# Second layer's up product by Strassen's seven half-block products, with weight factors made beside the first layer

## What is computed

```
    h = x @ w_in                       # layer one: 2304 x 512 times 512 x 2048
    r = np.maximum(h, 0.0)
    g = s * (r * r) + b
    x = (g @ w_out).astype(np.float32)
    ...
    h = x @ w_in                       # layer two, weights of its own
    g = np.maximum(h, 0.0) + alpha * np.minimum(h, 0.0)
    return (g @ w_out).astype(np.float32)
```

## Time and profile before

| | |
|---|---|
| median of 3 runs | 885.54 us (884.36 to 886.65) |
| the profiled execution, its time | 886.29 us |
| its span, first to last instruction | 884.0 us |
| PE busy | 870.4 us, 98% of the span |
| DVE / ACT / POOL busy | 416.4 / 289.2 / 55.8 us |
| matmuls of layer two | 1152 of 384 columns, 864 of 512 |
| mean granted TensorE clock | 0.996 |

### The profile page before, as it was taken

One profiled execution on the slowest core, in us unless ns is written; L12 is line 12 of the kernel. 1 busy time (PEld: TensorE's weight loads), 2 busy tenths in 40 slices (PEclk: granted clock), 3 DMA queues, 4 the chain that ended last, 5 costly groups with the idle time before them and its releaser, 6 DMA issues.

```text
span 884.0 us, 13811 instructions
## 1 busy us (share of the span) xinstructions
PE 870.4 (98%) x5628; PEld 816.5 (92%) x5628; DVE 416.4 (47%) x986; ACT 289.2 (33%) x727; POOL 55.8 (6%) x54
## 2 busy tenths in 40 slices
PE   6999999999999999999999999999999999999998
PEld 5899999999999999999999999999999999999997
DVE  6666544454444444443454444444444444444443
ACT  6566434344344344433554111111111111111111
POOL 4100000000000000000566000000000000000000
PEclk8999999999999999999999999999999999999999
DMA  7653311111121111201444001001100100100000
GB/s 251 215 161 101 118 60 53 55 66 55 55 66 62 41 55 67 72 1 64 128 127 145 15 1 42 30 1 33 39 1 27 47 0 19 54 1 7 30 1 36
DMA packets 19198, 53.05 MB, mean 60 GB/s; under 512 B 2112, under 2 KB 2112, under 8 KB 19136
## 3 DMA queue, kind: packets, MB, share of 16 engines
q1 hardware_dynamic: 19136, 52.18, 18.2%
HBM read 42.74 MB, written 9.44 MB: 59 GB/s over the span
## 4 chain that ended last, share of the span: by engine, by line
PE 93%; DVE 3%; ACT 3%; issue 0%; DMA 0%; DVEq 0%; ACTq 0%
PE hid L333 44%; PE acc L381 22%; PE acc L371 21%; PE bank_x L402 2%; PE bank_x L393 1%; ACT p L533 1%; PE bank_x L451 1%; PE bank_y L451 1%; ACT p L572 1%; ACT g L518 1%; DVE g L654 1%; DVE relu L640 1%; DVE w_in L664 0%; DVE p L738 0%; ACT w_in L528 0%
## 5 line engine op out<-in xcount | busy, mean ns | idle before, releaser
L333 PE MATMUL hid<-x,w_in 128*128 128x384 f32 (+1 forms) x2316 | 435.2, 336 | 0.0
L333 PEld LDWEIGHTS hid<-x,w_in 128*128 128x128 f32 x2316 | 406.0, 188 | 11.0 <-issue 2.6
L371 PE MATMUL acc<-g,w_out 128*128 128x384 f32 x1152 | 223.6, 337 | 1.1 <-DVE g L654 1.1
L381 PE MATMUL acc<-w_out,g 128*128 128x512 f32 x864 | 215.4, 393 | 0.4 <-DVE g L658 0.4
L371 PEld LDWEIGHTS acc<-g,w_out 128*128 128x128 f32 x1152 | 199.8, 188 | 2.8 <-DVE g L654 1.8
L381 PEld LDWEIGHTS acc<-w_out,g 128*128 128x128 f32 x864 | 160.7, 188 | 30.0 <-DVE g L658 0.8
L521 ACT ACTIVATE g<-relu 128x384 fp32r<-128x384 f32 x96 | 50.5, 526 | 332.2 <-DVE relu L648 332.2
L640 DVE SCALAR_TENSOR_TENSOR relu<-relu,consts 128x384 f32<-128x384 f32 x96 | 66.4, 692 | 152.3 <-ACT relu L508 152.3
L645 DVE TENSOR_SCALAR relu<-hid,consts 128x384 f32<-128x384 f32 x96 | 59.3, 618 | 161.5 <-PE hid L333 161.5
L508 ACT ACTIVATE relu<-hid 128x384 f32<-128x384 f32 x96 | 46.7, 486 | 130.6 <-PE hid L333 130.6
L654 DVE SCALAR_TENSOR_TENSOR g<-relu,consts,g 128x384 fp32r<-128x384 f32 x96 | 59.9, 624 | 57.4 <-ACT g L518 56.2
(11 more groups left out here) (85 smaller groups left out, 355.1 us busy)
## 6 DMA issues: line engine op xcount, KB each, us to landing
...
x_scratch<-outs SPq DMA_DIRECT2D x6, 768.0 KB, 4.1
qk<-x_scratch SPq DMA_DIRECT2D x6, 768.0 KB, 5.9
piece<-in_w_in_a SPq DMA_DIRECT2D x16, 256.0 KB, 2.6
piece<-in_w_out_a SPq DMA_DIRECT2D x16, 256.0 KB, 3.1
piece<-in_w_in_b SPq DMA_DIRECT2D x16, 256.0 KB, 2.8
piece<-in_w_out_b SPq DMA_DIRECT2D x16, 256.0 KB, 2.7
```

The costliest lines, as they stand in the source:

```text
L333: mm = pe.matmul(hid[f % 2][:, at], w_in[:, wi, f, dc, :], x[:, t % 2, xi, dc, at], start=(dc == 0 and n == 0), stop=(dc == ND - 1 and n = ...
L371: mm = pe.matmul(acc[dc][:, 0:TILE], w_out[:, wi, f, dc * 128:(dc + 1) * 128], g[:, f % 2, gi, :], start=(f == 0 and n == 0), stop=(f == N ...
L381: mm = pe.matmul(acc[a][:, :], g[:, f % 2, gi, a * 128:(a + 1) * 128], w_out[:, wi, f, :], start=(f == 0 and n == 0), stop=(f == NF - 1 an ...
```

## The change

Layer two's `up` is computed in passes. A pass k takes a tile of 768 tokens (two of the old ones) and two hidden blocks; there are 3 tiles of 8 passes (NW = 3, PER = 8, NK = 24). Width, tokens and hidden block pair are halved each, and the 8 half-block products become 7 (`multiply(k, n)`, line 494, 6 matmuls of 384 columns each), of sums of weight blocks (7 factors per hidden pair, `ring`) and sums of token blocks (7 per tile, `xc`). Their results are summed to the four quarters of the hidden values.

- **Weight factors.** Beside layer one, in tiles 1 to 4, in 14 of 16 steps: ACT makes a high part of 128 x 256 (`made_high`), DVE the low part (`made_low`) and in 8 of 14 a difference (`made_sum`); SP stores each factor (256 KB) to DRAM (`keep_made`). In layer two SP loads 7 a pass (`load_factor`, four slots) and ACT copies each into `ring` (`keep_factor`, line 740). POOL no longer splits layer two's `w_in`.
- **Token factors.** Once per tile: three sums and one more of 768 columns on DVE (`factor_sums`, `last_sum`), seven high parts on ACT (`factor_high`, line 718) and seven low parts on DVE (`factor_low`), 768 columns each.
- **A pass on DVE and ACT.** ACT copies product 0 (`copy_first`, 747). DVE has 7 `sum_up` (line 1050, PSUM plus SBUF), 4 `leak` of two instructions (lines 1059 and 1061, in SBUF now) and 4 `quarter_low` (line 1066); ACT has 4 `quarter_high` (line 756) and 7 `keep_factor`. All are 384 columns, the factor copies 2 x 256.
- **Down.** `gather(k, n)`, n = 0 to 5: 6 matmuls of 512 columns each, one of six 128-token blocks, as many as before. A pass of PE alternates `multiply(k, n)` with `gather(k - 1, n)` and ends with `multiply(k, 6)`. Output leaves by tile of 768 tokens, the last by block of 128.

The core of the diff:

```diff
+    PRODUCTS = (0, 2, 5, 1, 6, 4, 3)
+    QUARTERS = ((0, 0), (1, 0), (1, 1), (0, 1))
+    FACTOR_AT = (4, 5, 8, 9, 10, 11, 12)
+    FREED_BY_UP = {0: 1, 1: 3, 2: 4, 3: 6, 4: 7, 5: 9, 6: 10}
+    MADE = (0, 4, 1, 5, 2, 6, 3)
+    MADE_IN = (0, 0, 1, 0, 2, 0, 3)
+    NI = 7 * PER
+    LOADS = 4
...
-        w_in = sb("w_in", [128, 2, NF, ND, 128], F32R)
-        x = sb("x", [128, 2, 2, ND, TILE], F32R)
+        ring = [halves(at, 7 * 256).rearrange("p w (i n) -> p w i n", i=7) for at in (0, 14336)]
+        xc = [halves(3584 + 1536 * i, 2 * TILE) for i in range(7)]
...
+        def factor(i):
+            return (x2_in[:, 0], x2_in[:, 2], x2_in[:, 1], x2_in[:, 1], sums[:, 0], sums[:, 1], x2_in[:, 3])[i]
...
+            def keep_made(n):
+                sp.wait_ge(made_lo, n + 1)
+                sp.dma_start(factors[n // 7, MADE[n % 7]],
+                             made[:, n % 2].rearrange("p w n -> p (w n)")).then_inc(made_stored[n % 2], 16)
+            def load_factor(n):
+                k, at = divmod(n, 7)
+                if n == 0:
+                    sp.wait_ge(v_done, nth(NJ - 1))
+                    for b in range(2):
+                        sp.wait_ge(made_stored[b], 16 * NI // 2)
+                if n >= LOADS:
+                    sp.wait_ge(factor_kept, n - LOADS + 1)
+                sp.dma_start(loaded[:, n % LOADS].rearrange("p w n -> p (w n)"),
+                             factors[k % PER, PRODUCTS[at]]).then_inc(factor_here[n % LOADS], 16)
...
+            for n in range(LOADS):
+                load_factor(n)
+            store(NT - 2)
+            for n in range(LOADS, 7 + LOADS):
+                load_factor(n)
+            for n in range(NP + SLOTS, NP + NF):
+                load_piece(n)
...
+            def multiply(k, n):
+                tt, c = divmod(k, PER)
+                i = PRODUCTS[n]
+                pe.wait_ge(factor_kept, 7 * k + n + 1)
+                if c == 0:
+                    pe.wait_ge(xc_ready, 7 * tt + n + 1)
+                if k == 0 and n < 2:
+                    pe.wait_ge(hid_read, C_A)
+                elif n == 2:
+                    pe.wait_ge(copied, k + 1)
+                else:
+                    pe.wait_ge(summed, 7 * k + (-1, 0, 0, 1, 2, 3, 4)[n])
+                for cc in range(2):
+                    for m, (wi, xi) in enumerate(((0, 0), (0, 1), (1, 0))):
+                        mm = pe.matmul(hid[(7 * k + n) % 2][:, 0:TILE], ring[k % 2][:, wi, i, cc * 128:(cc + 1) * 128],
+                                       xc[i][:, xi, cc * TILE:(cc + 1) * TILE],
+                                       start=(cc == 0 and m == 0), stop=(cc == 1 and m == 2))
+                mm.then_inc(product, 1)
+            def gather(k, n):
+                tt, c = divmod(k, PER)
+                a = (n + NO) % NOB
+                if n == 0:
+                    pe.wait_ge(q_ready, 4 * k + 3)
+                if n == NO:
+                    pe.wait_ge(q_ready, 4 * k + 4)
+                if n == 0 and tt == 0:
+                    pe.wait_ge(*split_count(NP + 2 * c))
+                    pe.wait_ge(*split_count(NP + 2 * c + 1))
+                if c == 0 and tt == 0 and a < ND:
+                    acc_free(NT, a)
+                if c == 0 and tt > 0:
+                    pe.wait_ge(rows_act, NOB * (tt - 1) + n + 1)
+                for j in range(2):
+                    quarter = gq[k % 2][QUARTERS.index((a // NO, j))]
+                    for m, (gi, wi) in enumerate(((0, 0), (0, 1), (1, 0))):
+                        mm = pe.matmul(rows_bank[a][:, :], quarter[:, gi, a % NO * 128:(a % NO + 1) * 128],
+                                       w_out[:, wi, 2 * c + j, :], start=(c == 0 and j == 0 and m == 0),
+                                       stop=(c == PER - 1 and j == 1 and m == 2))
+                if c == PER - 1:
+                    mm.then_inc(rows_done, 1)
+                elif n == NOB - 1:
+                    mm.then_inc(pair_down, 1)
...
+                    up(c + LAG)
+            multiply(0, 0)
+            down(C_A - 2, 0)
+            multiply(0, 1)
+            down(C_A - 2, 1)
+            multiply(0, 2)
+            down(C_A - 1, 0)
+            multiply(0, 3)
+            down(C_A - 1, 1)
+            multiply(0, 4)
+            multiply(0, 5)
+            multiply(0, 6)
+            for k in range(1, NK):
+                for n in range(NOB):
+                    multiply(k, n)
+                    gather(k - 1, n)
+                multiply(k, NOB)
+            for n in range(NOB):
+                gather(NK - 1, n)
...
+            def keep_factor(n):
+                k, at = divmod(n, 7)
+                act.wait_ge(factor_here[n % LOADS], 16 * (n // LOADS + 1))
+                if k == 0:
+                    act.wait_ge(up_done, C_A - NF + 1)
+                elif k == 1:
+                    act.wait_ge(up_done, C_A - NF + 15)
+                else:
+                    act.wait_ge(product, 7 * (k - 1))
+                act.activation(ring[k % 2][:, :, PRODUCTS[at], :], loaded[:, n % LOADS], ACT.Copy).then_inc(factor_kept, 1)
+            def copy_first(k):
+                act.wait_ge(product, 7 * k + 1)
+                if k >= 1:
+                    act.wait_ge(summed, 7 * k - 2)
+                act.activation(partial[:, 0, :], hid[7 * k % 2][:, 0:TILE], ACT.Copy).then_inc(copied, 1)
+            def quarter_high(k, n):
+                act.wait_ge(h_active, 4 * k + n + 1)
+                if n == 0:
+                    if k < 2:
+                        act.wait_ge(down_done, C_A)
+                    else:
+                        pair_left(k - 2)
+                act.activation(gq[k % 2][n][:, 0, :], hidden[:, n % 2, :], ACT.Copy).then_inc(q_hi, 1)
...
+                if 1 <= t <= PER // 2 and i % 8:
+                    made_high(7 * (2 * (t - 1) + i // 8) + i % 8 - 1)
...
+            for k in range(NK):
+                tt, c = divmod(k, PER)
+                copy_first(k)
+                if tt < NW - 1 and c == PER - 1:
+                    factor_high(tt + 1, 0)
+                if tt > 0 and c == 0:
+                    factor_high(tt, 3)
+                    factor_high(tt, 4)
+                quarter_high(k, 0)
+                if k + 1 < NK:
+                    for n in range(4):
...
+                quarter_high(k, 1)
+                if k + 1 < NK:
+                    for n in range(4, 7):
+                        keep_factor(7 * (k + 1) + n)
+                if tt < NW - 1 and c == PER - 1:
+                    factor_high(tt + 1, 2)
...
+                quarter_high(k, 2)
+                quarter_high(k, 3)
...
-                    dve.tensor_scalar(relu[:, c % 2, :], hid[c % 2][:, 0:TILE], 0.0, alpha[:, f:f + 1],
-                                      ALU.min, ALU.mult).then_inc(negative, 1)
...
+            def made_sum(k, n):
+                if n == 0:
+                    dve.wait_ge(raw_here, 16 * (k + 1))
...
+            def made_low(n):
+                dve.wait_ge(made_hi, n + 1)
+                dve.tensor_tensor(made[:, n % 2, 1].bitcast(F32R), raw[:, MADE_IN[n % 7]], made[:, n % 2, 0],
+                                  ALU.subtract).then_inc(made_lo, 1)
+            def sum_up(k, n):
+                made_by, to, of = ((1, hidden[:, 0], partial[:, 0]), (2, partial[:, 1], partial[:, 0]),
+                                   (3, partial[:, 0], partial[:, 1]), (4, hidden[:, 1], partial[:, 0]),
+                                   (5, hidden[:, 0], partial[:, 0]), (5, partial[:, 1], partial[:, 1]),
+                                   (6, hidden[:, 1], partial[:, 1]))[n]
+                dve.wait_ge(product, 7 * k + made_by + 1)
+                if n < 2:
+                    dve.wait_ge(copied, k + 1)
+                if n >= 1:
+                    dve.wait_ge(summed, 7 * k + (0, 0, 2, 3, 3, 3, 6)[n])
+                if n in (0, 3) and k >= 1:
+                    dve.wait_ge(q_ready, 4 * k - 1 + n // 3)
+                elif n in (4, 6):
+                    dve.wait_ge(q_ready, 4 * k + n // 2 - 1)
+                dve.tensor_tensor(to, hid[(7 * k + made_by) % 2][:, 0:TILE], of, ALU.add).then_inc(summed, 1)
+            def leak(k, n):
+                f = 2 * (k % PER) + QUARTERS[n][1]
+                place = hidden[:, n % 2]
+                dve.wait_ge(summed, 7 * k + (1, 4, 5, 7)[n])
+                if k >= 1 or n >= 1:
+                    dve.wait_ge(h_active, 4 * k + n)
+                dve.tensor_scalar(below, place, 0.0, alpha[:, f:f + 1], ALU.min, ALU.mult).then_inc(h_below, 1)
+                dve.wait_ge(h_below, 4 * k + n + 1)
+                dve.scalar_tensor_tensor(out=place, in0=place, scalar=0.0, in1=below,
+                                         op0=ALU.max, op1=ALU.add).then_inc(h_active, 1)
+            def quarter_low(k, n):
+                dve.wait_ge(q_hi, 4 * k + n + 1)
```

(83 more changed lines are left out.)

387 lines of the change are left out of this document (243 added, 144 removed).

## The result

| | before | changed |
|---|---|---|
| median, run side by side | 886.1 us | 921.74 us (920.74 to 922.99) |
| ratio to before | | 1.040 [1.038, 1.043] |
| the profiled execution | 886.29 us | 921.57 us |
| its span; mean granted clock | 884.0 us; 0.996 | 919.8 us; 0.985 |
| forecast | | 907.5 us, range 898 to 921 |

The change makes the kernel 4.0% slower. The direction and the likeliest mechanism were forecast; the size was not: the predicted difference was +22.0 us on the profiled execution, the measured one is +35.3, and the time lies 0.7 us over the range. 13.3 us are to be explained.

A forecast was written before the change was run, and what follows sets the result against it. PE was taken as the bound, busy 870.4 of 884.0 us. Terms -25.3 + 30.8 + 5.8 + 7.9 + 1.8 + 1.0 = +22.0 on the profiled 886.3 gave 908.3, by the median 907.5 us; range 898 to 921.

The forecast's parts named there:

- six matmuls fewer, 24 passes: PE in layer two's passes: 42 matmuls of 384 columns in place of 48, -25.3 us while PE never waits.
- chain at a pass's end, 22 passes: Before gather(k, 0), PE waits for DVE's sums, leaks and quarter 2's low part: 1.4 us a pass, +30.8 us.
- tile ends: Passes 7 and 15: DVE's chain moves by 2.9 us behind ACT's factor copies and 768-column high part, +5.8 us.
- start of layer two: First products to gather(0, 0): waits for relu, copies, DVE's queue and factor loads behind a store, together +7.9 us.
- end: Last pass: no multiply covers its chain, so PE waits 2.45 us against 0.6 before, +1.8 us.
- layer one: Making 56 weight factors on ACT and DVE beside layer one loses little: +1 us, bounds 0 and 6.
- rival 2: PE's clock falls in pauses at start, both tile ends and end: four falls, +11 us, 918; chance 0.12.
- The min-and-scale: First half of DVE's leak, now from SBUF: estimated 0.42 us at two elements a step, bounds 0.25 and 0.62.
- Rival 1: DVE's min-and-scale from SBUF is as slow as from PSUM: 1.8 us a pass, 917 by the median; chance 0.17.
- Rival 3: Factor loads hold ACT up in layer two's passes: 0.5 us more lost a pass, 919; chance 0.05.
- Rival 4: DVE's queue from sum 4 to low part 2 is covered, no stall: 877; chance faster 0.07, within 0.3% 0.03.
- break-even point: At a pass's end: kernel breaks even at a stall of 0.4 us a pass, a chain of 3.6.

The follow-up runs named there:

- e2: Changed kernel with DVE's low part of quarter 2 moved ahead of product 6's sum and the last leak; 882.78 us, 0.9965 of the kernel before.
- e1: Changed kernel with DVE's low part of quarter 2 moved ahead of the last leak, behind sum 6; 894.13 us, 1.010 of the kernel before.
- e3: Changed kernel with ACT's third 768-column high part moved ahead of three factor copies at a tile's end; 911.41 us, 1.029 of the kernel before.
- e4: Changed kernel with SP's loads of factors 11 to 13 ahead of the store of layer one's last tile; 914.27 us, 1.033 of the kernel before.
- e6: Changed kernel with e5's and e4's edits, fewer waits at layer two's start, copies and sums spread in layer one's last tile; 861.59 us, 0.973 of before.
- e5: Changed kernel with the edits of e2 and e3 together; 874.80 us, 0.987 of the kernel before.

## Why the prediction was wrong in size and right in kind

| step | forecast | measured |
|---|---|---|
| six matmuls fewer, 24 passes | -25.3 | -26.4 (e2's 15.66 us a pass against 16.76) |
| chain at a pass's end, 22 passes | +30.8 | +33.3 (17.175 - 15.66 each) |
| tile ends | +5.8 | +5.8 |
| start of layer two | +7.9 | +10.6 |
| end | +1.8 | +1.8 |
| layer one | +1.0 | +3.5 |
| clock after the start and both tile ends | 0 (rival 2) | +7.0 |
| sum | +22.0 | +35.6, against 35.3 by the times and 35.8 by the spans |

**Right.** The min-and-scale, taken at 0.42 from a bound of 0.25 to 0.62, is 0.41 to 0.42 at line 1059: two elements a step. Rival 1 falls; on this operation the trace agrees with the Trainium skill ("VectorE: DVE Perf Modes", section on the perf-mode tier table). The overlaps of 0.08 and gaps of 0.03, read off other instructions, carry over: the chain came out 0.06 us long in nine of them. The first two steps together are 1.4 us over their forecast, most of it these 0.06 in 22 passes. (The idle time in a row is less than what the pass loses: 1.23 shown and 17.175 - 15.66 = 1.51 lost, in e1 0.18 shown and 0.43 lost.) Each tile end is 20.1 us long (605.35 to 625.44), 2.9 over a common pass, as worked out. Rival 3 falls: in common passes ACT never waits for a factor. Rival 4's mechanism is true, though it wasn't what the change did: e1 and e2 shorten the chain and the loss goes with it. Its break-even point, a stall of 0.4 a pass, rests on the other terms as forecast, and fell with them: e1 loses 0.43 a pass and is still 1% slower than before, because the start, layer one and the clock are not as forecast.

**Wrong, 7.0 us: the clock.** The step that failed is rival 2. It named the right places ("two pauses of 1.8 to 2.8 us with one group between"), had a row in which PE was almost without work for 3 us and the clock was at half after it, and priced a fall at 2.8 us. It then was held apart from the forecast as a rival of 0.12, and the sum had the clock at nothing. As the forecast itself contained the pauses, the falls were a consequence of it and belonged in its sum. Measured: +2.4 and +2.7 in the intervals after the two tile ends, +1.8 after the start. After the last gather's 2.27 there was none (e3 had one there, 0.58 in 896 to 900, after the same wait). Three falls at its own price of 2.8 would have made the forecast 916; without them the measured time would be near 915, inside the range. The rival's other half, the common pauses, was argued rightly: 1.00 there, also in e3.

**Wrong, 2.7 us: when the loads land.** The start's step had loads 11 on land "near 11.5", and ACT's quarter 2 behind them. With the store at 7.8 that is 3.7 us behind the store's issue: a load's 2.8 and little more, so the store cost its followers next to nothing, although the step names its 4.1. Here the store was issued at 491.73 and the first load at 492.10, and ACT could begin its copy only at 497.59, 5.9 us behind the store and 5.5 behind the load's own issue. The pause at `gather(0, 0)` is 5.83 for the 2.3 + 1.3 forecast: these 2.2 us are the step's error, and the other 0.5 lies in the start's smaller pauses. The store's median went from 4.1 to 5.7 us. e4 takes the store away from before the loads and gets 3.6 us back, so the order on SP is the cause; what within the queues made it 5.5 is not settled.

**Wrong, 2.5 us: layer one.** My "+1, bounds 0 and 6" priced the making of the factors and assumed that nothing was lost where ACT and DVE had room. Making them cost 0.15 us (PE is 1.20 behind the kernel before near 35 us, and 1.35 at 427). What cost was a part that I had not costed at all, in the last tile: four and three factor copies in two steps on ACT, behind loads still under way, which delay the relu ahead of the first wait below; and three sums of 768 columns at one place on DVE, ahead of the second. PE's waits there:

```profile
434.25 2.37 PE L473 MATMUL acc<-split_mem,w_out 128*128 128x384 f32 x12 [0.48 <-DVE split_mem L890]
...
435.10 1.94 DVE L1002 TENSOR_TENSOR plain_mem<-plain_mem 128x768 f32<-128x768 f32 x1
...
439.78 2.38 PE L473 MATMUL acc<-split_mem,w_out 128*128 128x384 f32 x12 [1.08 <-DVE split_mem L890]
```

That is 1.6 us of pauses, and with the restarts 2.15 us of time; e6 spreads the copies over seven steps and the sums over three, and has neither pause. The other 1.2 us arose in the opening (PE's wait at 34.74 before stood at 35.94). The same wait stands at 34.61 to 35.29 in e1 to e5 and at 32.99 in e6, whose edits don't touch the opening, so these 1.2 us can't be put down to the change. The clock's fall there differs too: from 24 to 28 us 0.67 was granted in the changed kernel's profiled execution and 1.00 in the kernel before's.
